# Loading the first quarter of w_in in two pairs at the attention's load steps 16 and 17, in place of one part in each of the steps 13 to 16

## What is computed

```python
# attention, for each batch and head
q_d, k_d, v_d = means of q, k, v over groups of 4 tokens        # 144 pooled tokens
out_d = softmax(q_d @ k_d.T / 8) @ v_d                          # pooled part
out_local = softmax(where(|i-j| < 4, q @ k.T / 8, -1e9)) @ v    # local band
x = repeat(out_d, 4) + out_local
x = x as (2304, 512)
# first layer
h = x @ w_in          # 512 -> 2048
x = (h * tanh(softplus(h))) @ w_out
# second layer
h = x @ w_in2         # 512 -> 1024
solu = h * softmax(h)
out = (layernorm(solu) * g_ln) @ w_out2
```

## Time and profile before

| | value |
|---|---|
| three executions | 688.67, 689.77, 690.86 us |
| span of the profiled execution | 686.9 us |
| TensorE matmuls | 667.5 us busy, 97% of the span |
| VectorE | 425.9 us, 62% |
| ScalarE | 326.0 us, 47% |
| GpSimd | 284.2 us, 41% |
| mean granted TensorE clock | 0.995 |
| loads and stores | 37.52 MB |

### The profile page before, as it was taken

The page is one execution under the profiler, slowest core; times in us unless marked ns, Lnnn a source line. Parts: engine busy times, 40 slices in busy tenths (PEclk is TensorE's granted clock), DMA queues, the critical chain, the costliest instruction groups (busy, mean ns, idle before and its releaser), DMA issues.

```text
span 686.9 us, 12938 instructions
## 1 busy us (share of the span) xinstructions
PE 667.5 (97%) x5002; PEld 573.1 (83%) x5002; DVE 425.9 (62%) x747; ACT 326.0 (47%) x687; POOL 284.2 (41%) x342
## 2 busy tenths in 40 slices
PE   6998899999999999999999999999999999999998
PEld 5777778888999989989899988888778888888886
DVE  7998759555765557555544412555788566766671
ACT  5998773233543446543443211137464454535441
POOL 6999713020694636645000000576435543354100
PEclk9999999999999999999999999999999999999999
DMA  8999692000000000000100001012100000000001
GB/s 259 247 262 262 157 336 114 0 1 1 0 1 1 1 1 1 1 1 1 62 1 2 1 0 35 27 31 63 31 17 16 31 32 31 8 25 31 32 16 46
DMA packets 26085, 37.52 MB, mean 55 GB/s; under 512 B 2484, under 2 KB 12714, under 8 KB 26026
## 3 DMA queue, kind: packets, MB, share of 16 engines
q1 hardware_dynamic: 26026, 36.71, 18.0%
HBM read 31.98 MB, written 4.72 MB: 53 GB/s over the span
## 4 chain that ended last, share of the span: by engine, by line
PE 89%; POOL 3%; DVE 2%; issue 2%; ACT 1%; DMA 1%; SPq 0%; POOLq 0%; DVEq 0%
PE psum L961 29%; PE psum L913 16%; PE psum L1074 13%; PE psum L1051 12%; PE psum L947 12%; PE psum L1060 2%; PE psum L813 1%; POOL prob L676 1%; PE psum L845 1%; PE psum L893 1%; DVE so L1768 1%; PE psum L832 1%; POOL half_qk L649 1%; DMA qkT<-kT_dram 1%; POOL half_v L659 1%
## 5 line engine op out<-in xcount | busy, mean ns | idle before, releaser
L961 PE MATMUL psum<-ghi,whi 128*128 128x512 f32 (+1 forms) x320 | 118.2, 370 | 0.0
L961 PE MATMUL psum<-glo,whi 128*128 128x512 f32 (+1 forms) x320 | 118.1, 369 | 0.0
L961 PE MATMUL psum<-ghi,wlo 128*128 128x512 f32 (+1 forms) x320 | 117.7, 368 | 0.0
L1210 ACT ACTIVATE g_sb<-psum 128x512 f32<-128x512 f32 (+1 forms) x48 | 25.3, 527 | 135.5 <-PE psum L913 134.7
L1586 DVE CAST ghi<-g_sb 128x512 fp32r<-128x512 f32 (+1 forms) x48 | 24.0, 500 | 101.8 <-PE psum L961 86.7
L913 PE MATMUL psum<-xhi,whi 128*128 128x512 f32 (+1 forms) x256 | 85.6, 365 | 0.5 <-ACT g_sb L1210 0.3
L1591 DVE TENSOR_TENSOR glo<-g_sb,ghi 128x512 fp32r<-128x512 f32 (+1 forms) x80 | 66.3, 829 | 19.6 <-ACT ghi L1236 17.9
L961 PEld LDWEIGHTS psum<-ghi,wlo 128*128 128x128 f32 x320 | 60.3, 189 | 10.2
L961 PEld LDWEIGHTS psum<-ghi,whi 128*128 128x128 f32 x320 | 60.5, 189 | 9.8 <-issue 0.4
L913 PE MATMUL psum<-xlo,whi 128*128 128x512 f32 (+1 forms) x192 | 68.0, 354 | 0.0
L961 PEld LDWEIGHTS psum<-glo,whi 128*128 128x128 f32 x320 | 60.5, 189 | 8.9
(11 more groups left out here) (175 smaller groups left out, 1618.7 us busy)
## 6 DMA issues: line engine op xcount, KB each, us to landing
wraw<-w_dram SPq DMA_DIRECT2D x12, 512.0 KB, 7.5
vw<-v_dram SPq DMA_DIRECT2D x30, 160.0 KB
qkT<-qT_dram SPq DMA_DIRECT2D x16, 288.0 KB, 4.0
qkT<-kT_dram SPq DMA_DIRECT2D x16, 288.0 KB, 5.7
out_dram<-ob SPq DMA_DIRECT2D x18, 256.0 KB, 2.0
v<-v_dram SPq DMA_DIRECT2D x16, 256.0 KB, 5.8
wraw<-w_dram SPq DMA_DIRECT2D x16, 256.0 KB, 6.8
b<-w_dram SPq DMA_DIRECT2D x4, 512.0 KB, 4.3
```

The source lines that it names most:

```text
L961: ins = nc.tensor.matmul(psum[:, YB + m, 0:size], a[:, w], b[:, (t * F1 + f) % GR, 0:size], start=(f == 0 and n == 0), stop=(f == F1 - 1 a ...
L1210: nc.scalar.activation(g_sb[:, f % HR, 0:size], psum[:, HB1 + f % HB, 0:size], ACT.Mish).then_inc(g_ok, 1)
```

## The change

The tuple W_IN holds for each of the four parts of the first quarter the load step in which it is issued. Before, it was looked up by step and each step could have one part. After, a loop over the parts issues each whose step has come. The parts 0 and 1 are issued at the end of step 16, the parts 2 and 3 at the end of step 17. Sources, sizes, destinations, semaphores and all other instructions stay.

```diff
-        W_IN = (13, 14, 15, 16)
+        W_IN = (16, 16, 17, 17)
...
                 if s > 2:
                     load_windows(s - 3)
-                if s in W_IN:
-                    load_w_in(0, W_IN.index(s))
+                for kdx in range(KD):
+                    if s == W_IN[kdx]:
+                        load_w_in(0, kdx)
```

## The result

The changed kernel is slower by 0.4%: its median over 15 runs is 691.67 us, that of the kernel before 688.67 us over 15 runs, and the ratio is 1.0042 (95% interval 1.0029 to 1.0056), which is 2.9 us (2.0 to 3.9). One execution of all that follow, of the kernel with all parts in step 16, took 1101.54 us at a mean granted clock of 0.56, and is in no ratio.

What follows compares the result with a forecast made beforehand. TensorE, busy for 97% of the span, was taken as the bound, with the attention's last units touched. Landing +0.2 us and clock +1.4 us summed to +1.6 us, taking 689.77 to 691.4 us, range 689.5 to 693.7.

Steps and rivals of the forecast that it cites:

- The gain of lighter loads: Attention before 73 us: three of four parts leave the queue; direct gain 0, as no attention load was effectively waited for.
- The new wait on ScalarE for the second pair: weights_in_high(0) waits for parts 2 and 3, issued behind load_windows(14): 3.5 to 4.5 us, ending at 82.1 to 82.6.
- TensorE waited 4.61 us at value_pooled(13): Sign: TensorE should wait some 3.7 us for copy_pooled, with granted clock 0.50 for about 3 us behind it.
- The distance: Sign: the delay with which hidden(0, 0) starts, 1.0 to 1.6 us, should be kept to the end.
- hidden(0, 0) would start 1.0 to 1.6 us later: Sign on TensorE: hidden(0, 0) should start some 1.0 to 1.6 us later than 86.19.
- The clock: A 1.2 GHz spell moves onto value_pooled(13) to hidden(0, 0): 1.4 us lost, ends 0 and 1.7.
- The landing: The pair issued behind the windows lands 3.4 us after issue, at 82.1, or 82.6 if the windows' transfers hold it.
- The gap: TensorE's 2.41 us gap in value_local(12) at 76.28, read as late instructions behind data, goes: 2.4 us, ends 0 and 2.41.
- the sum: +0.2 us (landing against end of scores) plus 1.4 us (clock) gives +1.6 us, so 689.77 becomes 691.4.
- +0.2 predicted: TensorE's value_pooled(13) starts at 83.35 to 83.85 in place of 83.47: -0.1 to +0.4 us, taken as +0.2.
- The second case: Gap stays, last part lands at 84.5, value_pooled(13) starts at 85.8: +2.3 to +4.0 us, 692.1 to 693.8; chance 0.34.
- The likeliest case: Gap goes, the load wait replaces it, the clock spell moves onto bound work: 690.9 to 691.9 us; chance 0.53.

Runs made afterwards that it cites:

- the parts early: Kernel before with the four parts issued in steps 6, 7, 8 and 9 (W_IN = (6, 7, 8, 9)): 688.57 us against 689.3, ratio 0.9991.
- weights_in_high(0) later: Changed kernel with weights_in_high(0) moved on ScalarE from the end of iteration 14 to just ahead of weights_in_high(1) in iteration 15: 688.59 us, ratio 0.9990.
- the light queue: Value windows of units 4 to 14 cut to one of five per half, values stale: kernel before 685.29 us, changed kernel 690.46 us.

## Why the prediction was right, and which of its steps were not

**The place and the mechanism** were right. The gain of lighter loads, apart from the gap, was put at 0, and the kernel with the parts early agrees. The new wait on ScalarE for the second pair, behind load_windows(14), took 5.56 us where 3.5 to 4.5 were said; it ended at 82.5, where 82.1 to 82.6 were said. TensorE waited 4.61 us at value_pooled(13), where 3.7 were said, and the slow clock fell on work that nothing else bounded. The distance was kept to the end. The kernels with all parts in step 16 and in step 17 show the dependence on the landing, and the one with weights_in_high(0) later shows that it works through ScalarE's order.

**That hidden(0, 0) would start 1.0 to 1.6 us later was too little.** It was 2.38 us. Two terms were mis-sized, and one hid an error:

- The clock: 1.4 us was taken, with 1.7 as the upper end, from the time that the scores lost in the spell of rows 7. Measured, the group from value_pooled(13) to hidden(0, 0) loses 2.2 us and hidden(0, 0) 0.3. The spell was longer: 0.50 from 82.1 to 89.0 us, 6.8 us and not 3.4, and all of it behind 83.7 met bound work. The end of 1.7 rested on taking the length of one spell for a fixed one.
- The landing: 3.4 us was taken from rows 5, 4.2 us was measured. The second issue of the pair took 1.72 us itself, where 0.61 was assumed, on a queue that was not as empty as at 86.77.
- The gap: I took it for an effect of the queue, made worse by w_in, that would vanish with three parts fewer. The first half holds: with the light queue it is gone. The second doesn't. It was 1.11 us in the changed kernel, and with weights_in_high(0) later a gap of 3.27 us came at 28.7 us, 47 us ahead of the first part of w_in. So in the kernel before it wasn't a cost that the change could remove, but one draw of many. I subtracted 2.4 us of it in the sum and compared with a profile that held all of it. In the two profiles this came out at value_pooled(13) as +0.25 us against +0.2 predicted, by luck: the changed execution was 1.45 us ahead already, kept 1.11 us of the gap, and took 0.5 us more from the end of value_local(12) to value_pooled(13) (7.44 against 83.67 - 76.74 = 6.93).

The second case, in which the gap stays, was put at +2.3 to +4.0 us; its mechanism was the gap at its old size, which isn't what happened, but its arithmetic is that of a change that wins nothing back from the gap. The measured +2.9 us lies in it. The likeliest case should have counted the gap as a mean over executions, the same on both sides. That the time itself came out within 0.3 us is luck too: the difference was 1.3 us short, and the three runs of the kernel before that it was added to stood 1.1 us above fifteen.

**Still open** is why the full kernels differ by 2.9 us (3.3 in the group of the light ones) and the light ones by 5.2. The heavy queue costs the full kernel before 3.3 us and the changed kernel 691.9 - 690.46 = 1.4 us in the same comparison, so the change seems to win back some 1.9 us, with a spread of the runs of about 1 us either way. The wait may swallow gaps that would have come later; a gap late in the attention brings a slow clock of its own in the kernel before (1.2 us in its profile), while in the changed kernel the slow clock comes anyway; or the queue without w_in may make fewer gaps. No run tells these apart. It also bears on the kernel with weights_in_high(0) later: its median is that of the kernel before though 3.1 us are left in its profile.

## What to carry to other kernels

A load issued behind a wait pays that wait, the issues ahead of it and its landing in full, and the engine that waits for it stops everything queued behind, here copies that had nothing to do with the load; moving the waiting instruction behind them brought the median back to that of the kernel before, and took 3 of the 6 us away by the profiles. If the wait stops TensorE for some microseconds, add the slow clock behind it, which was two fifths of this loss. To compare single profiles, count from a mark just ahead of the place that changed. And a gap in one profile without a semaphore behind it should be looked for at the same instruction count in another profile before it is put into a sum.

## What the runs showed of the hardware that was not expected

TensorE stood still for up to 3.5 us at fixed counts of its instructions, about 250 apart, when the DMA share was near 1.00, and in three profiles not once behind 30 us when it was 0.70 to 0.72. Each gap of 1 us or more ended 2.6 to 2.9 us after the start of a 16 KB packet of instructions. The gap of the kernel with the parts early, in TensorE's timeline:

```profile
54.24 0.51 PE L833 MATMUL psum<-qkT 64*64 64x64 f32 x18 [3.50 <-issue]
```

A float32 matmul of 128x128 with 64 columns runs as two passes of 0.114 us. A part of 256 KB took 3.0 us to land on the light queue, 4.2 us behind the windows in the changed kernel, and up to 8.7 us in the full one. The granted clock fell to 0.50 in each of the five waits of 3.7 to 6.2 us of TensorE, and stayed there for 6.8 us each time. Shorter stops went either way: 2.41 us in the kernel before was followed by 3.4 us at 0.50, and 1.67 us with weights_in_high(0) later too, but a gap of 2.47 us in the kernel with all parts in step 17 was not:

```profile
42.57 0.81 PE L833 MATMUL psum<-qkT 64*64 64x64 f32 x38 [2.47 <-issue]
...
40.00:46.00 6.00, 3.53 (x101) 2.90 (x99) 3.38 (x7) 3.56 (x12) 4.31 (x6) 1.00 0.90 202
```
